# The values of the folded stage's attention blocks, two at a time instead of one by one

## The chip, the cores and the metric

The kernel runs on one core of a Trainium2 chip. A core has five engines, each with its own instruction stream: TensorE (PE in the profile), VectorE (DVE), ScalarE (ACT), GpSimd (POOL) and SyncE (SP), which here only issues loads. They meet through semaphores. The metric is the device time of one execution in microseconds, the median over the runs.

## The reference

Three stages follow each other. The first is attention over a window of 64 positions, for 4 batches, 8 heads, 576 positions and a head dimension of 64:

```python
scores = scale * np.matmul(q, k.transpose(0, 1, 3, 2))
mask = (rel >= 0) & (rel < window)
scores = np.where(mask, scores, -1000000000.0)
attn = np.exp(scores - np.max(scores, axis=-1, keepdims=True))
attn = attn / (np.sum(attn, axis=-1, keepdims=True) + 1e-09)
return np.matmul(attn, v).astype(np.float32)
```

The second is a gated product, the third a mixture of 8 experts of which each token takes the one with the largest logit:

```python
h = a * b @ w3                      # a = x @ w1, b = x @ w2
x = h @ w_out
h = np.maximum(x[mask] @ w1[e], 0.0)
out[mask] = gate_w[mask, None] * eom[mask, e, None] * (h @ w2[e])
```

## The kernel before

Products in full precision are made of three matmuls of a high and a low part of each operand (`product3`): ScalarE writes the high part of a tile, VectorE the low part, which is the difference.

**The fold.** Before any token is worked on, the kernel multiplies `w3` by `w_out` (with the gate weights beside it) into one matrix, `Wh` and `Wl`. That takes 16 steps, in the order of `w_order`. Each is 24 matmuls of 128 x 256 or 128 x 272 into one of banks 0 to 3 of PSUM. Then ScalarE copies the bank into `Wh` and VectorE puts the rest into `Wl`. The steps are numbered by `i` from 0 to 15. The code for attention counts `e = i - 2`.

**Attention blocks.** Attention is cut into blocks of three times 64 positions for four heads. The stage here called `b = 0` is the first four blocks, `p` = 0 to 3, and it is worked on between the steps of the fold. The others (`b > 0`) are worked on in the main loop, four in each chunk of 384 tokens, between its tiles. A block passes through this chain:

- `score` (TensorE, L593): 12 matmuls.
- `masks` (VectorE): scale and mask, lay out into `prob`, row maximum.
- `exps` (ScalarE): exponentials and their sums, in `prob`.
- `weigh` (VectorE) and `normal` (GpSimd, L1474): reciprocal of the sums, multiplication of `prob`. It releases `p_ok`.
- `turn` (TensorE, L609): three transposes of `prob` into a bank. It releases `pt_done`.
- `turn_out` (VectorE, L1055): four instructions for a block that copy the transposes into `pT` with the mask at the sides. They release `pt_ok`, two for a block.
- `value` (TensorE, L621): 12 matmuls of `vv` and `pT` into a bank. It releases `o_done`.
- `value_hi` (ScalarE, L850) and `value_lo` (VectorE, L1069): the result as high and low part in `xTh` and `xTl`. `value_lo` releases `o_lo`.

`prob` has two buffers and `pT` four, of which a block uses two (`buf_of`). Loads of values go into two buffers as well, and `load_v(G)` on SyncE's queue waits until block G - 2 has been multiplied (`o_done`).

**What sets the order.** Each engine runs its instructions in the order in which the program gives them. The tables `scored`, `laid`, `raised`, `weighed`, `turned` and `valued` say at which `e` a part of a block's work stands; on TensorE, `attend` puts it behind the matmuls of that step, as turns, values, scores. On VectorE a step has first its own part (`own`: weights' low parts and the step's `Wl`), then turned, valued, laid. `last_valued` are the blocks whose values stand in the middle of the last step, after its third group of matmuls. The first chunk begins when `o_lo` has counted all four blocks.

Of the kernel before, what the change touches and what calls it, by code (L numbers as in the profile page):

```python
# [37 lines left out]
def build(nc, B, H, S, qk_pairs, v_pairs, w1, w2, w3T_in, w_out, w_outT, w_gates, ew1, ew2, out):  # L38
# [35 lines left out]
    NP = len(PLACES) // STAGES  # L74
# [7 lines left out]
    with ctx:  # L82
# [131 lines left out]
        bank = [ctx.enter_context(nc.psum_tensor(f"bank{i}", [P, 512], F32)) for i in range(8)]  # L214

        def sem(name):
            return ctx.enter_context(nc.semaphore(name))
# [19 lines left out]
        pt_done, pt_ok, o_done, o_hi, o_lo = sem("pt_done"), sem("pt_ok"), sem("o_done"), sem("o_hi"), sem("o_lo")  # L237
# [31 lines left out]

        head_of_row = lambda G: PLACES[G][2] == 0  # L270
        score_bank = lambda b, p, h: bank[(4 if b > 0 and p == 1 else 5) + 2 * h]
        turn_bank = lambda b, p: bank[6 if b > 0 and p % 2 else 4]
        value_bank = lambda b, p: bank[4 if b > 0 and p % 2 else 6]
        buf_of = lambda p, h: p % 2 * 2 + h
        stats = lambda p: slice(p % 2 * 6, p % 2 * 6 + 6)

# [11 lines left out]
            return ({2: (0,), 3: (1,), 7: (2,), 9: (3,)} if b > 0 else {2: (0,), 4: (1,), 7: (2,), 10: (3,)}).get(e, ())  # L288

        def turned(b, e):  # L290
            return ({3: (0,), 4: (1,), 9: (2,), 11: (3,)} if b > 0 else {4: (0,), 7: (1,), 9: (2,), 11: (3,)}).get(e, ())

        def valued(b, e):
            return ({6: (0, 1)} if b > 0 else {7: (0,), 9: (1,), 11: (2,)}).get(e, ())

        def last_valued(b):
            return (2, 3) if b > 0 else (3,)

# [23 lines left out]
        def hidden_bank(cc, f, m):  # L324
            return bank[(2 * (cc + f) + m) % 4]
# [159 lines left out]
        def _(pe):  # L485
# [112 lines left out]

            def turn(b, p):
                G = b * NP + p  # L600
                if b == 0 and G > 0:
                    pe.wait_ge(pt_ok, 2 * G)
                if b > 0 and p < 2:
                    pe.wait_ge(masked, 2 * (b * NP + 2))
                if b > 0 and p >= 2:
                    pe.wait_ge(o_lo, b * NP + 2)
                pe.wait_ge(p_ok, G + 1)
                for i in range(3):
                    mm = pe.transpose(turn_bank(b, p)[:, i * P:(i + 1) * P], prob[p % 2][:, i * P:(i + 1) * P], ident[:, :])  # L609
                mm.then_inc(pt_done, 1)  # L610

            def value(b, p):
                G = b * NP + p
                pe.wait_ge(v_in[G % 2], 16 * (G // 2 + 1))
                pe.wait_ge(pt_ok, 2 * G + 2 if b == 0 else 2 * (b * NP + p // 2 * 2 + 2))
                if b == 0 and G > 0:
                    pe.wait_ge(o_lo, G)
                for h in range(2):
                    for i in range(3):
                        for r in range(2):  # L620
                            mm = pe.matmul(value_bank(b, p)[r * D:(r + 1) * D, (3 * h + i) * WIN:(3 * h + i + 1) * WIN],  # L621
                                           vv[G % 2][:, (i * 4 + r * 2 + h) * D:(i * 4 + r * 2 + h + 1) * D],
                                           pT[buf_of(p, h)][:, i * P + r * WIN:i * P + (r + 1) * WIN], start=True, stop=True)
                mm.then_inc(o_done, 1)
# [11 lines left out]
            for i, (it, n) in enumerate(w_order):  # L636
                if i == 0:
                    W_first_two()
                if i < 2:
                    continue  # L640
                def between(j):
                    if (i, j) == (2, 4):
                        pe.wait_ge(wg_in, 16)
                        G1_product(0)
                    if (i, j) in ((3, 0), (3, 1), (3, 3)):
                        G1_product((j + 3) // 2)
                    if (i, j) == (3, 6):
                        pe.wait_ge(const_ok, 1)
                        G1_turn()
                    if (i, j) == (len(w_order) - 1, 2):  # L650
                        for p in last_valued(0):
                            value(0, p)

                W_half(it, n, between)
                if i < len(w_order) - 1:
                    attend(0, i - 2)

            def chunk(cc, c, b, final):
                pe.wait_ge(o_lo, (cc + 1) * NP)
                pe.wait_ge(xB_ok, cc * CT + 1)  # L660
                pe.wait_ge(xA_ok, max(cc * CT - 1, 1))

                def hidden_tile(f):
                    if f < 2:
                        pe.wait_ge(W_lo, 2 * KF - 2 + 2 * f)
                        if f == 1 and cc > 0:
                            pe.wait_ge(xA_ok, cc * CT + 1)
                    else:
                        pe.wait_ge(a_ok, cc * KF + (f - 1))
                        pe.wait_ge(ab_ok, cc * KF + (f - 1))  # L670
                    for m, (wh, wl, done) in enumerate(((w1h, w1l, a_done), (w2h, w2l, b_done))):
                        for kt in range(KD):
                            if cc == 0 and f == 0:
                                pe.wait_ge(w12_lo, m * KD + kt + 1)
                            ws = slice(kt * FF + f * P, kt * FF + (f + 1) * P)
                            xc = slice(kt * SUPER + c * CH, kt * SUPER + (c + 1) * CH)
                            mm = product3(hidden_bank(cc, f, m)[:, 0:CH], wh[:, ws], wl[:, ws], xTh[:, xc], xTl[:, xc],
                                          kt == 0, kt == KD - 1)
                        mm.then_inc(done, 1)

                def row_tile(i, n, tt, between=None):
                    if i == 0:
                        pe.wait_ge(a_ok, cc * KF + (KF - 1))
                        pe.wait_ge(ab_ok, cc * KF + (KF - 1))
                    if i >= 4:
                        pe.wait_ge(xB_ok, cc * CT + (i - 2))
                    first, end = PARTS[n]
                    for f in range(KF):
                        if i == 0:
                            pe.wait_ge(ab_lo, cc * KF + (f + 1))  # L690
                        ts = slice(f * CH + tt * P, f * CH + (tt + 1) * P)
                        ws = slice(f * WXC + first, f * WXC + end)
                        mm = product3(row_bank(cc, i)[:, 0:end - first], abh[:, ts], abl[:, ts], Wh[:, ws], Wl[:, ws],
                                      f == 0, f == KF - 1)
                        if between and f == 2:
                            between()
                    mm.then_inc((xA_done, xB_done)[n], 1)

                if b is not None:
                    score(b, 0)  # L700
                    score(b, 1)
                for f in range(KF):
                    hidden_tile(f)
                    if b is not None:
                        attend(b, f)
                    if final and f == 1:
                        early_ranks()
                    if final and f == 4:
                        early_ids()
                for n, tt, i in row_tiles:  # L710
                    if b is not None and KF + i == NSTEP - 1:
                        row_tile(i, n, tt, lambda: [value(b, p) for p in last_valued(b)])
                    else:
                        row_tile(i, n, tt)
                        if b is not None:
                            attend(b, KF + i)
                    if final and i == 1:
                        x_transposes(0, bank[7])
                    if final and i == CT:
                        last_ranks()  # L720
# [115 lines left out]
        def _(act):  # L836
# [47 lines left out]
            for i, (it, n) in enumerate(w_order):  # L884
# [10 lines left out]
                                   ACT.Copy).then_inc(W_hi, 1)  # L895

                if i == len(w_order) - 1:
                    for p in last_valued(0):
                        value_hi(0, p)
                own()  # L900
                for p in valued(0, i - 2):
# [16 lines left out]
            def chunk(cc, c, b, final):  # L918
# [27 lines left out]
                                xs_out(0, bank[7])  # L946
                for n, tt, i in row_tiles:
                    if b is not None and KF + i == NSTEP - 1:
                        for p in last_valued(b):
                            value_hi(b, p)  # L950
                    row_tile(i, n, tt)
                    attend(KF + i)
# [76 lines left out]
        def _(dve):  # L1029
# [88 lines left out]
            for i, (it, n) in enumerate(w_order):  # L1118
# [25 lines left out]
                    dve.tensor_tensor(Wl[:, ws], w_bank(i)[:, 0:end - first], f32(Wh[:, ws]), ALU.subtract).then_inc(W_lo, 1)  # L1144

                if i == len(w_order) - 1:
                    for p in last_valued(0):
                        value_lo(0, p)
                own()
                attend(0, i - 2)  # L1150
# [8 lines left out]
            def chunk(cc, c, b, final):  # L1159
# [32 lines left out]
                for n, tt, i in row_tiles:  # L1192
# [4 lines left out]
                        else:  # L1197
                            xs_out(0, bank[7])
                    if b is not None and KF + i == NSTEP - 1:
                        for p in last_valued(b):  # L1200
                            value_lo(b, p)
                    row_tile(i, n, tt)
                    if b is not None:
# [389 lines left out]
```

## Time and profile before

| | |
|---|---|
| median of 3 runs | 697.99 us (697.89 to 698.15) |
| the profiled execution | 697.63 us, span 695.5 us |
| TensorE busy | 688.3 us, 99% of the span |
| VectorE busy | 367.7 us, 53% |
| ScalarE busy | 269.0 us, 39% |
| GpSimd busy | 105.9 us, 15% |
| the fold on TensorE | about 5.6 to 67.3 us |

The busy times are those of one execution, whose times in the rows count from the start of its span. The span leaves out what lies around it, about 2 us. The shares are averages over stages that differ: over the whole span VectorE has much room, but from 40 to 50 us it is busy for 9.77 of 10 us.

### The profile page before, as it was taken

What the parts mean: (1) busy time and instruction counts of PE and PEld (TensorE: products, weight loads), DVE (VectorE), ACT (ScalarE), POOL (GpSimd) and SP (SyncE); (2) the same over time, 40 slices, a digit from 0 to 9 for tenths busy, and PEclk for the clock granted to TensorE, in tenths of its full rate; (3) what the DMA queues carried; (4) which work ended last, traced back from release to release, by engine and by line L of the source; (5) the groups of instructions that cost most, each with busy time, mean ns of one, the idle gap of its engine ahead of it and who ended that gap; (6) DMA issues with size and microseconds to landing.
All of it is one profiled execution on the core that took longest, in us unless ns stands there. A gap on an engine that the chain in (4) does not pass through costs nothing.

```text
span 695.5 us, 14656 instructions
## 1 busy us (share of the span) xinstructions
PE 688.3 (99%) x5043; PEld 629.2 (90%) x5044; DVE 367.7 (53%) x696; ACT 269.0 (39%) x653; POOL 105.9 (15%) x173
## 2 busy tenths in 40 slices
PE   8999999999999999999999999999999999999997
PEld 6899999999999999999999998888888888888885
DVE  5598565355265546436535488654465634652111
ACT  5546432234143232324322255263454535542121
POOL 7110001000000100000010002222222222221111
PEclk9999999999999999999999999999999999999999
DMA  8973112302402030240125053844456554411110
GB/s 330 341 252 109 50 41 75 130 27 73 142 4 99 33 113 27 73 146 1 47 88 200 16 182 135 282 162 155 161 179 228 190 166 161 151 36 45 33 45 31
DMA packets 29917, 82.76 MB, mean 119 GB/s; under 512 B 3565, under 2 KB 3693, under 8 KB 29872
## 3 DMA queue, kind: packets, MB, share of 16 engines
q1 hardware_dynamic: 24832, 66.66, 28.1%
q0 software_dynamic: 5040, 15.47, 6.4%
q8 instruction: 32, 0.52, 0.3%
q14 instruction: 13, 0.11, 0.0%
HBM read 72.68 MB, written 10.49 MB: 120 GB/s over the span
## 4 chain that ended last, share of the span: by engine, by line
PE 96%; DMA 2%; SPq 1%; issue 0%; POOLq 0%; ACT 0%; ACTq 0%
PE bank L489 29%; PE bank L491 28%; PE bank L490 28%; PE bank L786 3%; PE bank L621 3%; PE bank L593 3%; DMA qk<-in_qk 2%; PE bank L764 1%; PE bank L609 1%; PE bank L746 1%; SPq L403 1%; SPq L390 0%; SPq L399 0%; PE bank L741 0%; POOLq L82 0%
## 5 line engine op out<-in xcount | busy, mean ns | idle before, releaser
L489 PE MATMUL bank<-Wh,abh 128*128 128x272 f32 (+1 forms) x288 | 83.5, 290 | 0.0
L491 PE MATMUL bank<-Wh,abl 128*128 128x272 f32 (+1 forms) x288 | 82.0, 285 | 0.0
L1156 DVE TENSOR_TENSOR wbuf<-raw,wbuf 128x1024 f32 (+1 forms) x64 | 75.3, 1221 | 12.5 <-ACT wbuf L915 12.4
L490 PE MATMUL bank<-Wl,abh 128*128 128x272 f32 (+1 forms) x288 | 81.7, 284 | 0.0
L1350 DVE TENSOR_TENSOR hTl<-bank,hTh 128x512 fp32r<-128x512 f32 x44 | 28.4, 686 | 97.3 <-ACT hTh L965 97.3
L1169 DVE TENSOR_TENSOR ab_f<-bank,a_sb 128x384 f32<-128x384 f32 x48 | 26.8, 558 | 90.5 <-PE bank L491 90.0
L489 PE MATMUL bank<-wbuf,hTh 128*128 (+1 forms) x176 | 70.7, 402 | 0.0
L489 PE MATMUL bank<-wbuf,xsTh 128*128 (+1 forms) x176 | 70.4, 400 | 0.0
L491 PE MATMUL bank<-wbuf,hTl 128*128 (+1 forms) x176 | 68.8, 391 | 0.0
L491 PE MATMUL bank<-wbuf,xsTl 128*128 (+1 forms) x176 | 68.6, 390 | 0.0
L490 PE MATMUL bank<-wbuf,xsTh 128*128 (+1 forms) x176 | 68.6, 390 | 0.0
L490 PE MATMUL bank<-wbuf,hTh 128*128 (+1 forms) x176 | 68.5, 389 | 0.0
L489 PE MATMUL bank<-xTh,w1h 128*128 128x384 f32 x192 | 66.5, 346 | 0.0
L491 PE MATMUL bank<-xTh,w1l 128*128 128x384 f32 x192 | 64.3, 335 | 0.0
L490 PE MATMUL bank<-xTl,w1h 128*128 128x384 f32 x192 | 64.3, 335 | 0.0
L491 PE MATMUL bank<-xTh,w2l 128*128 128x384 f32 x192 | 64.2, 334 | 0.0
L489 PE MATMUL bank<-xTh,w2h 128*128 128x384 f32 x192 | 64.1, 334 | 0.0
L490 PE MATMUL bank<-xTl,w2h 128*128 128x384 f32 x192 | 64.1, 334 | 0.0
L915 ACT ACTIVATE wbuf<-raw 128x1024 f32 (+1 forms) x64 | 64.0, 1054 | 0.0
L923 ACT ACTIVATE abh<-ab_f 128x384 fp32r<-128x384 f32 x48 | 25.2, 525 | 98.2 <-DVE ab_f L1169 98.2
L1474 POOL TENSOR_TENSOR prob<-prob,rec 128x384 f32<-128x384 f32 x24 | 21.7, 905 | 257.0 <-DVE rec L1065 257.0
L1055 DVE TENSOR_TENSOR pT<-bank,side 64x384 f32<-64x384 f32 x96 | 52.8, 550 | 14.6 <-PE bank L609 13.2
(208 smaller groups left out, 1438.1 us busy)
## 6 DMA issues: line engine op xcount, KB each, us to landing
raw<-in_expert_w SPq DMA_DIRECT2D x64, 512.0 KB, 4.4
qk<-in_qk SPq DMA_DIRECT2D x24, 448.0 KB, 4.3
vv<-in_v SPq DMA_DIRECT2D x24, 384.0 KB, 4.0
x_rows<-x_sb POOLq DMA_DIRECT2D x18, 256.0 KB, 2.3
w3r<-in_w3T SPq DMA_DIRECT2D x5, 512.0 KB, 3.6
wo<-in_w_out SPq DMA_DIRECT2D x8, 256.0 KB, 8.2
woT<-in_w_outT SPq DMA_DIRECT2D x4, 512.0 KB, 8.6
w1r<-in_w SPq DMA_DIRECT2D x4, 512.0 KB, 4.8
```

What stands on the lines that cost most here:

```text
L489: pe.matmul(dst, lh, rh, start=first, stop=False)
L490: pe.matmul(dst, lh, rl, start=False, stop=False)
L491: return pe.matmul(dst, ll, rh, start=False, stop=last)
L593: mm = pe.matmul(score_bank(b, p, h)[r * WIN:(r + 1) * WIN, i * P:(i + 1) * P], buf[rows, r * QC + i * WIN:r * QC + (i + 1) * WIN], buf[ro ...
L621: mm = pe.matmul(value_bank(b, p)[r * D:(r + 1) * D, (3 * h + i) * WIN:(3 * h + i + 1) * WIN], vv[G % 2][:, (i * 4 + r * 2 + h) * D:(i * 4 ...
L915: act.activation(wbuf[:, bass.ds(wcol(e, part, 0, c * PC), PC)], raw[part * NP1 + c][:, :], ACT.Copy).then_inc(ew_hi[part], 1)
L923: act.activation(abh[:, f * CH:(f + 1) * CH], ab_f[f % 2][:, :], ACT.Copy).then_inc(ab_hi, 1)
L1055: cut = dve.tensor_tensor(pT[buf_of(p, h)][w * WIN:(w + 1) * WIN, :].rearrange("p (i r c) -> p i r c", r=2, c=WIN), turn_bank(b, p)[rows, ...
L1156: dve.tensor_tensor(wbuf[:, bass.ds(wcol(e, part, 1, c * PC), PC)], raw[part * NP1 + c][:, :], f32(wbuf[:, bass.ds(wcol(e, part, 0, c * PC ...
L1169: dve.tensor_tensor(ab_f[f % 2][:, :], hidden_bank(cc, f, 1)[:, 0:CH], a_sb[f % 2][:, :], ALU.mult).then_inc(ab_ok, 1)
L1350: dve.tensor_tensor(hTl[last][:, cols], bank[3 + n][:, :], f32(hTh[last][:, cols]), ALU.subtract).then_inc(hT_lo, 1)
L1474: pool.tensor_tensor(pv, pv, rec[:, stats(p)].unsqueeze(2).broadcast_to([P, 6, WIN]), ALU.mult).then_inc(p_ok, 1)
```

## The change

The values of blocks 0 and 1 are both multiplied behind step 9 (`e` = 7), those of blocks 2 and 3 both in the last step. Before, they stood behind step 9, 11 and 13 and in the last step. The transposes of block 1 stand behind step 8 instead of 9. The banks of odd blocks are exchanged: their transposes go to bank 6 and their values to bank 4, as in the main loop. With that the waits change: `value` waits for the `pt_ok` of both blocks of its pair, and `turn` of blocks 2 and 3 waits for the `o_lo` of blocks 0 and 1.

```diff
-        turn_bank = lambda b, p: bank[6 if b > 0 and p % 2 else 4]
-        value_bank = lambda b, p: bank[4 if b > 0 and p % 2 else 6]
+        turn_bank = lambda b, p: bank[6 if p % 2 else 4]
+        value_bank = lambda b, p: bank[4 if p % 2 else 6]
...
         def turned(b, e):
-            return ({3: (0,), 4: (1,), 9: (2,), 11: (3,)} if b > 0 else {4: (0,), 7: (1,), 9: (2,), 11: (3,)}).get(e, ())
+            return ({3: (0,), 4: (1,), 9: (2,), 11: (3,)} if b > 0 else {4: (0,), 6: (1,), 9: (2,), 11: (3,)}).get(e, ())
 
         def valued(b, e):
-            return ({6: (0, 1)} if b > 0 else {7: (0,), 9: (1,), 11: (2,)}).get(e, ())
-
-        def last_valued(b):
-            return (2, 3) if b > 0 else (3,)
+            return {6 if b > 0 else 7: (0, 1)}.get(e, ())
+
+        last_valued = (2, 3)
...
             def turn(b, p):
                 G = b * NP + p
-                if b == 0 and G > 0:
-                    pe.wait_ge(pt_ok, 2 * G)
                 if b > 0 and p < 2:
                     pe.wait_ge(masked, 2 * (b * NP + 2))
-                if b > 0 and p >= 2:
+                if p >= 2:
                     pe.wait_ge(o_lo, b * NP + 2)
...
                 pe.wait_ge(v_in[G % 2], 16 * (G // 2 + 1))
-                pe.wait_ge(pt_ok, 2 * G + 2 if b == 0 else 2 * (b * NP + p // 2 * 2 + 2))
-                if b == 0 and G > 0:
-                    pe.wait_ge(o_lo, G)
+                pe.wait_ge(pt_ok, 2 * (b * NP + p // 2 * 2 + 2))
```

The other places of the diff take `last_valued` as a tuple instead of calling it.

TensorE at the end of step 9, before. The first row is the step's last matmul; `prob1` is block 1's probabilities, `pT0` and `pT1` are block 0's transposes.

```order
L491 MATMUL bank1<-xTl_56,w3l0_106 128x272
L609 MATMUL bank4<-ident_81,prob1_72 128x128 [waits p_ok,pt_ok]
L609 MATMUL bank4<-ident_81,prob1_72 128x128 x2
L621 MATMUL bank6<-pT0_73,vv0_68 64x64 [waits pt_ok,v_in0]
L621 MATMUL bank6<-pT0_73,vv0_68 64x64 x5
L621 MATMUL bank6<-pT1_74,vv0_68 64x64 x6
L593 MATMUL bank5<-qk1_67 64x128 [waits masked,qk_in1]
```

The same place after. `pT2` and `pT3` are block 1's transposes, `vv1` its values.

```order
L490 MATMUL bank1<-xTl_56,w3l0_106 128x272
L616 MATMUL bank6<-pT0_73,vv0_68 64x64 [waits pt_ok,v_in0]
L616 MATMUL bank6<-pT0_73,vv0_68 64x64 x5
L616 MATMUL bank6<-pT1_74,vv0_68 64x64 x6
L616 MATMUL bank4<-pT2_75,vv1_69 64x64 [waits pt_ok,v_in1]
L616 MATMUL bank4<-pT2_75,vv1_69 64x64 x5
L616 MATMUL bank4<-pT3_76,vv1_69 64x64 x6
L592 MATMUL bank5<-qk1_67 64x128 [waits masked,qk_in1]
```

Block 1's transposes have left this place and its values have come to it; the first values' `pt_ok` now counts both blocks. The transposes stand between step 8 and step 9, as follows (after):

```order
L490 MATMUL bank0<-xTl_56,w3l0_106 128x256
L606 MATMUL bank6<-ident_81,prob1_72 128x128 [waits p_ok]
L606 MATMUL bank6<-ident_81,prob1_72 128x128 x2
L488 MATMUL bank1<-xTh_55,w3h0_110 128x272 [waits g1_lo,W_lo,w3_lo]
```

VectorE around the same steps, before. The rows begin with the two low parts of weights and the `Wl` of step 8 (out of bank 0); the `Wl` out of bank 1 is that of step 9.

```order
L1076 TENSOR_TENSOR w3l2_108<-w3r2_104,w3h2_112 128x1024 [waits w3_hi]
L1083 TENSOR_TENSOR w1l_50<-w1r_115,w1h_49 128x1024 [waits w12_hi]
L1144 TENSOR_TENSOR Wl_54<-bank0,Wh_53 128x256 [waits W_hi]
L1063 TENSOR_SCALAR sums_85<-sums_85 128x6 [waits exp_ok]
L1065 RECIPROCAL rec_86<-sums_85 128x6 [waits sum_ok]
L1144 TENSOR_TENSOR Wl_54<-bank1,Wh_53 128x272 [waits W_hi]
L1055 TENSOR_TENSOR pT2_75<-bank4,side_78 64x384 [waits pt_done]
L1055 TENSOR_TENSOR pT2_75<-bank4,side_78 64x384
L1055 TENSOR_TENSOR pT3_76<-bank4,side_78 64x384 [waits pt_done]
L1055 TENSOR_TENSOR pT3_76<-bank4,side_78 64x384
L1069 TENSOR_TENSOR xTl_56<-bank6,xTh_55 128x2x192 [waits o_hi]
```

And after:

```order
L1071 TENSOR_TENSOR w3l2_108<-w3r2_104,w3h2_112 128x1024 [waits w3_hi]
L1078 TENSOR_TENSOR w1l_50<-w1r_115,w1h_49 128x1024 [waits w12_hi]
L1139 TENSOR_TENSOR Wl_54<-bank0,Wh_53 128x256 [waits W_hi]
L1050 TENSOR_TENSOR pT2_75<-bank6,side_78 64x384 [waits pt_done]
L1050 TENSOR_TENSOR pT2_75<-bank6,side_78 64x384
L1050 TENSOR_TENSOR pT3_76<-bank6,side_78 64x384 [waits pt_done]
L1050 TENSOR_TENSOR pT3_76<-bank6,side_78 64x384
L1058 TENSOR_SCALAR sums_85<-sums_85 128x6 [waits exp_ok]
L1060 RECIPROCAL rec_86<-sums_85 128x6 [waits sum_ok]
L1139 TENSOR_TENSOR Wl_54<-bank1,Wh_53 128x272 [waits W_hi]
L1064 TENSOR_TENSOR xTl_56<-bank6,xTh_55 128x2x192 [waits o_hi]
L1064 TENSOR_TENSOR xTl_56<-bank4,xTh_55 128x2x192 [waits o_hi]
```

The four copies of block 1's transposes have moved up past the sums of block 2 and past step 9's `Wl`, three instructions; what stands ahead of them is as before. The low part of block 1's values has come up from the next step but one.

## Rows read from the trace of the kernel before

**Rows 1.** The page, busy time of the engines, with share of the span and instructions.

```profile
PE 688.3 (99%) x5043; PEld 629.2 (90%) x5044; DVE 367.7 (53%) x696; ACT 269.0 (39%) x653; POOL 105.9 (15%) x173
```

**Rows 2.** TensorE's waits over the span: total us, times, longest.

```profile
PE bank L577 <- DVE prob L1099: 1.5, 1, 1.5
PE bank L593 <- DMA qk<-in_qk: 1.0, 2, 0.6
```

**Rows 3.** Timeline of TensorE in the fold: start, us, instructions merged.

```profile
43.61 0.29 PE L491 MATMUL bank<-xTl,w3l 128*128 128x272 f32 x1
43.73 0.49 PE L609 MATMUL bank<-ident,prob 128*128 128x128 f32 x3
44.16 0.92 PE L621 MATMUL bank<-pT,vv 128*64 128x64 f32 x24
45.00 0.89 PE L593 MATMUL bank<-qk 64*64 64x128 f32 x24
45.82 0.39 PE L489 MATMUL bank<-xTh,w3h 128*128 128x256 f32 x1
...
58.98 0.49 PE L609 MATMUL bank<-ident,prob 128*128 128x128 f32 x3
...
60.25 0.39 PE L489 MATMUL bank<-xTh,w3h 128*128 128x256 f32 x1
...
64.41 0.92 PE L621 MATMUL bank<-pT,vv 128*64 128x64 f32 x24
65.26 0.39 PE L489 MATMUL bank<-xTh,w3h 128*128 128x272 f32 x1
```

**Rows 4.** Timeline of TensorE in two chunks of the main loop.

```profile
112.56 0.49 PE L609 MATMUL bank<-ident,prob 128*128 128x128 f32 x3
112.81 0.37 PE L489 MATMUL bank<-Wh,abh 128*128 128x272 f32 x1
...
182.02 0.28 PE L491 MATMUL bank<-Wh,abl 128*128 128x256 f32 x1
182.22 1.62 PE L621 MATMUL bank<-pT,vv 128*64 128x64 f32 x48
183.77 0.38 PE L489 MATMUL bank<-Wh,abh 128*128 128x256 f32 x1
```

**Rows 5.** Timeline of VectorE in the fold.

```profile
40.65 1.01 DVE L1037 SCALAR_TENSOR_TENSOR sm<-bank,mask 128x384 f32<-128x384 f32 x2
...
42.76 1.22 DVE L1076 TENSOR_TENSOR w3l<-w3r,w3h 128x1024 fp32r<-128x1024 f32 x1
43.90 1.22 DVE L1083 TENSOR_TENSOR w1l<-w1r,w1h 128x1024 fp32r<-128x1024 f32 x1
45.03 0.42 DVE L1144 TENSOR_TENSOR Wl<-bank,Wh 128x256 fp32r<-128x256 f32 x1
45.36 0.16 DVE L1063 TENSOR_SCALAR sums<-sums 128x6 f32<-128x6 f32 x1
...
45.98 2.27 DVE L1055 TENSOR_TENSOR pT<-bank,side 64x384 f32<-64x384 f32 x4
```

**Rows 6.** Timelines of GpSimd and ScalarE in the fold; in brackets the idle time before.

```profile
35.43 1.73 POOL L1474 TENSOR_TENSOR prob<-prob,rec 128x384 f32<-128x384 f32 x1 [8.27 <-DVE rec L1065]
...
57.09 1.72 POOL L1474 TENSOR_TENSOR prob<-prob,rec 128x384 f32<-128x384 f32 x1 [10.42 <-DVE rec L1065]
...
53.15 0.49 ACT L850 ACTIVATE xTh<-bank 128x384 fp32r<-128x384 f32 x1 [0.79 <-PE bank L621]
```

**Rows 7.** TensorE's first and last matmuls, and a window with granted clock (PEclk).

```profile
5.60 0.77 PE L541 MATMUL bank<-xTh,w3h 128*128 128x256 f32 x2
...
8.00 0.40 PE L541 MATMUL bank<-xTh,w3h 128*128 128x256 f32 x2
...
690.40 0.39 PE L491 MATMUL bank<-wbuf,hTl 128*128 x1
...
692.00:694.00 2.00, 0.00 (x0) 0.00 (x0) 0.00 (x0) 0.00 (x0) 0.98 (x1) 0.75 0.03 12
```

More of the change, by code:

```diff
@@ L650, in between @@
                     if (i, j) == (len(w_order) - 1, 2):
-                        for p in last_valued(0):
+                        for p in last_valued:
                             value(0, p)
@@ L711, in chunk @@
                     if b is not None and KF + i == NSTEP - 1:
-                        row_tile(i, n, tt, lambda: [value(b, p) for p in last_valued(b)])
+                        row_tile(i, n, tt, lambda: [value(b, p) for p in last_valued])
                     else:
@@ L897, in _ @@
                 if i == len(w_order) - 1:
-                    for p in last_valued(0):
+                    for p in last_valued:
                         value_hi(0, p)
@@ L948, in chunk @@
                     if b is not None and KF + i == NSTEP - 1:
-                        for p in last_valued(b):
+                        for p in last_valued:
                             value_hi(b, p)
@@ L1146, in _ @@
                 if i == len(w_order) - 1:
-                    for p in last_valued(0):
+                    for p in last_valued:
                         value_lo(0, p)
@@ L1199, in chunk @@
                     if b is not None and KF + i == NSTEP - 1:
-                        for p in last_valued(b):
+                        for p in last_valued:
                             value_lo(b, p)
```

## The prediction

> **What bounds the kernel now.** I read the page first: TensorE is busy for 99% of the span [rows 1], so time is won or lost only where TensorE's own stream gets shorter or where it has to stand still. The view of waits then says how rarely it stands: 1.5 us before the first matmul and 1.0 us for two loads of queries and keys [rows 2], and nothing at all between those loads and the end of the fold. Every microsecond of waiting that the change puts into the fold therefore goes into the total, because nothing later is idle that could give it back.
>
> Next, TensorE's timeline at the places where attention work interrupts the fold. I write T for the three transposes of a block (L609), V for its values (L621), S for its scores (L593). What counts is from start to start: from the first instruction of the interruption to the next fold matmul. Step 9 ends in T, V, S of blocks 1, 0, 3: T begins at 43.73, V at 44.16, S at 45.00, the fold goes on at 45.82, so T V S costs 2.09 us, of which S is 0.82. Step 13 ends in T V, 58.98 to 60.25, 1.27 us, and step 11 in the same. The V in the last step runs from 64.41 to 65.26, 0.85 us [rows 3]. Then VectorE's timeline just ahead of step 9's end: it hands one instruction to the next without a gap from 40.65 to 45.98 [rows 5]. In this stretch VectorE is as much as two steps behind TensorE: its share of step 8, the low part of the folded matrix, starts at 45.03, when TensorE is already through step 9.
>
> **The change part by part.** *The interruptions.* The chunks of the main loop already take the new forms, so their prices are in the trace: T alone costs 0.25 us (112.56 to 112.81), and two V's together 1.55 us (182.22 to 183.77), behind a lead of 0.20 us where 0.12 is usual (43.61 to 43.73), 0.08 more [rows 3, 4]. Before: 2.09 + 1.27 + 1.27 + (0.85 + 0.08) = 5.56 us. After: T behind step 8 0.25, V V S behind step 9 0.08 + 1.55 + 0.82 = 2.45, T behind steps 11 and 13 0.25 each, V V in the last step 1.63, together 4.83 us. The arrangement saves 0.73 us of TensorE's time. The work is the same; what goes is changes between kinds of matmuls.
>
> The Trainium skill (TensorEngine Tiling (Array Packing), its list of constraints) says that a change of the tiling mode drains TensorE. The saving above has that sign, and by that rule alone the change would be a small gain.
>
> *T of block 1, one step sooner.* Its probabilities are ready: GpSimd's multiplication for it starts at 35.43 and takes 1.73 us, to 37.16 [rows 6], and step 8 ends near 40.7 (step 9's 24 matmuls, 0.12 us apart, end at 43.73). So T itself waits for nothing.
>
> *V of block 0, now with block 1.* Its wait on `pt_ok` was for block 0 alone; now it is for both blocks. Block 1's transposes are copied out by VectorE in four instructions of together 2.27 us [rows 5]. In VectorE's order these now stand right behind the low part of step 8 and ahead of the two small operations at 45.36 and of step 9's low part. What is ahead of them is unchanged and has no gap: scores' mask at 40.65, two splits at 42.76 and 43.90, the low part at 45.03, next start 45.36 [rows 5]. None of it waits for TensorE's later work, so moving T forward does not make VectorE come sooner. The copies run from 45.36 to 45.36 + 2.27 = 47.63. TensorE is ready for V V at 43.73 + 0.25 (the T put in behind step 8) + 0.08 = 44.06. It waits 47.63 − 44.06 = 3.57 us. Before, V of block 0 needed only copies that were long done, and block 1's copies were covered by two more steps, 10 and 11. That cover is gone. Queued behind the waiting V on TensorE are V of block 1, S of block 3 and all of steps 10 to 15, and every other engine ends up waiting for these.
>
> Sum of the fold: 3.57 − 0.73 = +2.84 us.
>
> *What is late next.* T of block 2 now waits for both low parts of the values (`o_lo`), which VectorE does some 2.5 us after V V begins; two whole steps lie between. T of block 3 is the closest one: now its probabilities are ready at 57.09 + 1.72 = 58.81, and T starts at 58.98, 0.17 us later [rows 3, 6]. After the change T of block 3 comes 3.57 + (0.25 + 2.45 − 2.09) − (1.27 − 0.25) = 3.16 us later. The chain to the probabilities starts from step 11's end, later by 3.57 + 0.61 = 4.18, but ScalarE loses the copy of block 1's values from it, 0.79 us of waiting and some 0.4 us of work [rows 6]; that makes about 3.0. The margin stays, thin. I cost it at nothing, with up to 1 us as its bad end. V V in the last step wants block 3's copies, 2.3 us of VectorE behind T; there the last V came five microseconds behind T and V V comes one microsecond sooner, so some margin is left. The loads of values are issued in pairs now; the one that moves later is used in the middle of the first chunk, tens of microseconds on. Nothing.
>
> *The clock of TensorE after the wait.* No row of before shows a wait like this inside the kernel. The nearest rows: the last matmul starts at 690.40 and takes 0.39 us, and the granted clock averages 0.75 in 692 to 694, half of it at 2.4 GHz and half at 1.2; it fell about 2.2 us after the last matmul [rows 7]. A wait of 3.57 us is longer than that, so I expect the lower level behind it. What that costs is bounded by the beginning: from the first matmul at 1.5 us [rows 2], two 256-column matmuls still take 0.77 us at 5.60 and only 0.40 us at 8.00 [rows 7] (the clock record itself reads 1.00 there; the durations say half). So the return took 4.1 to 6.5 us, and half of that, 2.0 to 3.2 us, is lost. Below, the bound is 0, if the clock doesn't fall or is back at once. I take the middle of 0 to 3.2, 1.6 us.
>
> The Trainium skill (TensorE: Matmul & The Clock Gate, "What's actually happening") says that the lower clock is the default and that activity lifts it. By that rule a stall is paid for twice, which is the term that I add; without it the sum would be 1.6 us less.
>
> Total: 2.84 + 1.6 = +4.44 us. The profiled execution took 697.63 us (span 695.5), which gives 702.1; the median of the runs is 0.36 us above it, which gives 697.99 + 4.44 = **702.4 us**.
>
> **The rivals.**
> *The wait without the clock.* Same stall, clock stays at 2.4 GHz: 697.99 + 2.84 = 700.8 us. For it: after the last matmul the clock held for 2.2 us, and when it falls may differ from place to place. Against it: the wait is longer by more than a microsecond. 22%.
> *VectorE is in time (the other side).* Then only the regrouping counts: 697.99 − 0.73 = 697.3 us, not slower. It needs the copies to start by 44.06 − 2.27 = 41.8 us, 3.6 us sooner than 45.36; this decides it. For it only that ScalarE and the loads might release VectorE's earlier work sooner; against it, the chain in [rows 5] has no gap from 40.65 on that could close. 6%.
> *A shorter wait.* The copies start partly sooner, TensorE waits some 2 us or less and keeps its clock: 697.99 + 2 − 0.73 = 699.3 us. 5%.
> *More than one wait, or a long stay at the low clock.* The probabilities of block 3 are late as well, by up to 1 us, or the low clock costs its full 3.2 us: 703.4 to 704.0 us, both together 705.0. The margin of 0.17 us speaks for it, the shorter chain on ScalarE against it. 9%.
>
> **How the numbers follow.** My forecast, the wait with the clock's fall at about 1.6 us, has 58%. With the wait alone (22%) that is 80%; the range from 700.3 to 703.9 us takes in both, the clock term's spread and nearly all of the long stay. A measurement of this kernel tells about 0.2% (1.4 us) from no change. Faster by more than that needs a mechanism that no row shows: 2%. Within it lie VectorE in time and a part of the shorter wait: 8%. Slower: 90%.
>
> **What the profile after would show.** In VectorE's timeline the four copies at about 45.4 to 47.6, ahead of the sums of block 2. In the view of waits a line of TensorE's V waiting for VectorE's pT, about 3.6 us, once; this is the step on which all rests. V V behind step 9 and in the last step at about 1.55 us each, if the clock is up; behind step 9 nearer to 3 us, and the next fold matmuls 0.21 to 0.25 us apart in place of 0.12, if it fell; the granted clock of 48 to 52 us well below 1. T of block 3 without a wait. The first chunk starting about 4.4 us later (2.8 if the clock held), and from there the same distance between all rows of before and after. I am wrong if VectorE reaches the copies early, if the clock stays up, or if a second wait shows in steps 12 to 15.

## The result, and the profile after

The changed kernel takes 702.58 us (median of 6 runs, 701.9 to 704.15) beside 697.94 us (median of 6, 697.38 to 698.2) for the kernel before: ratio 1.0072, 95% interval 1.0061 to 1.0082. It is 4.64 us slower. The profiled execution took 702.89 us with a span of 700.8 us. Three executions in all that follows ran far slower than every other of their kernel (879.93 and 973.4 us of the kernel before, 1380.4 us in one experiment); they are left out of the ratios and move the medians below by at most 0.07 us.

Busy time, share and instructions by engine, after, from the page:

```profile
PE 689.2 (98%) x5043; PEld 630.1 (90%) x5044; DVE 368.7 (53%) x696; ACT 269.2 (38%) x653; POOL 105.9 (15%) x173
```

The work is that of [rows 1]; only the span around it is longer. TensorE's waits over the span, after (total us, times, longest):

```profile
PE bank L616 <- DVE pT L1050: 3.5, 1, 3.5
PE bank L592 <- DMA qk<-in_qk: 1.6, 2, 1.3
PE bank L576 <- DVE prob L1094: 1.5, 1, 1.5
```

The first line is new; the other two are those of [rows 2], the loads' with 0.6 us more in this execution. TensorE's values wait once, for the copies of the transposes. Its timeline there, after, from the T behind step 8 to the end of step 10, and further below T V V S in the rest of the fold (L606 is T, L616 V, L592 S, L488 to L490 the fold):

```profile
41.39 0.49 PE L606 MATMUL bank<-ident,prob 128*128 128x128 f32 x3
41.63 0.37 PE L488 MATMUL bank<-xTh,w3h 128*128 128x272 f32 x1
...
44.59 0.28 PE L490 MATMUL bank<-xTl,w3l 128*128 128x272 f32 x1
48.41 1.76 PE L616 MATMUL bank<-pT,vv 128*64 128x64 f32 x48 [3.54 <-DVE pT L1050]
50.10 1.56 PE L592 MATMUL bank<-qk 64*64 64x128 f32 x24
51.59 0.58 PE L488 MATMUL bank<-xTh,w3h 128*128 128x256 f32 x1
...
52.19 0.41 PE L490 MATMUL bank<-xTh,w3l 128*128 128x256 f32 x1
52.40 0.41 PE L488 MATMUL bank<-xTh,w3h 128*128 128x256 f32 x1
...
53.34 0.28 PE L490 MATMUL bank<-xTh,w3l 128*128 128x256 f32 x1
53.46 0.28 PE L488 MATMUL bank<-xTh,w3h 128*128 128x256 f32 x1
...
55.21 0.29 PE L488 MATMUL bank<-xTh,w3h 128*128 128x272 f32 x1
...
58.47 0.36 PE L488 MATMUL bank<-xTh,w3h 128*128 128x256 f32 x1
...
61.41 0.29 PE L488 MATMUL bank<-xTh,w3h 128*128 128x272 f32 x1
...
64.43 0.49 PE L606 MATMUL bank<-ident,prob 128*128 128x128 f32 x3
64.67 0.36 PE L488 MATMUL bank<-xTh,w3h 128*128 128x256 f32 x1
...
68.84 1.62 PE L616 MATMUL bank<-pT,vv 128*64 128x64 f32 x48
70.39 0.39 PE L488 MATMUL bank<-xTh,w3h 128*128 128x272 f32 x1
```

VectorE in the same stretch, after:

```profile
41.29 1.01 DVE L1032 SCALAR_TENSOR_TENSOR sm<-bank,mask 128x384 f32<-128x384 f32 x2
...
43.40 1.22 DVE L1071 TENSOR_TENSOR w3l<-w3r,w3h 128x1024 fp32r<-128x1024 f32 x1
44.53 1.22 DVE L1078 TENSOR_TENSOR w1l<-w1r,w1h 128x1024 fp32r<-128x1024 f32 x1
45.67 0.42 DVE L1139 TENSOR_TENSOR Wl<-bank,Wh 128x256 fp32r<-128x256 f32 x1
46.00 2.27 DVE L1050 TENSOR_TENSOR pT<-bank,side 64x384 f32<-64x384 f32 x4
48.30 0.17 DVE L1058 TENSOR_SCALAR sums<-sums 128x6 f32<-128x6 f32 x1
```

And the engines' busy times and granted clock (PEclk, third number from the end) in windows, after:

```profile
46.00:48.00 2.00, 0.00 (x0) 0.00 (x0) 1.94 (x5) 0.00 (x0) 0.00 (x0) 1.00 0.66 242
48.00:50.00 2.00, 1.58 (x48) 1.60 (x48) 1.18 (x5) 0.49 (x1) 0.83 (x1) 0.94 0.00 0
50.00:52.00 2.00, 2.00 (x29) 1.57 (x27) 1.26 (x3) 1.44 (x2) 0.00 (x0) 0.50 0.68 197
52.00:54.00 2.00, 2.00 (x14) 2.00 (x14) 0.97 (x1) 0.00 (x0) 0.00 (x0) 0.71 0.58 159
```

How to read these against the rows of before. VectorE does the same work in the same order up to 45.67, as in [rows 5], only 0.64 us later, because the fold itself began later behind the loads. From 46.00 to 48.27 it copies block 1's transposes. TensorE could have begun the pair at 44.59 + 0.20 = 44.79 and begins it at 48.41: 3.62 us. Then the pair takes 1.69 us (48.41 to 50.10) where it takes 1.55 in [rows 4], the scores 1.49 (50.10 to 51.59) where they took 0.82 in [rows 3], and step 10 takes 3.62 (51.59 to 55.21) where step 12, of the same 24 matmuls, takes 2.94 (58.47 to 61.41). That is 0.14 + 0.67 + 0.68 = 1.49 us for the clock. It is still at 2.4 GHz through the wait and for the first 1.3 us of the pair, then at 1.2 GHz from about 49.7 to about 53.2. The sum: 3.62 + 1.49 − 0.73 = 4.38 us, and with 0.6 us more for the loads 5.0 of the 5.3 us by which the two spans differ. The first chunk starts at 73.94 us where it started at 68.82, 5.1 us later, and the last matmul at 695.66 instead of 690.40, 5.3 us later: nothing behind the fold gave time back.

### The profile page after: what moved, and what is told of

Same layout as the page of the kernel before. It is cut to its first block, busy times and chain, and to the rows that moved or that the text cites. A ratio compares the mean times of both kernels' runs of the same rounds, so it can differ in the third digit from the quotient of the medians.

```text
span 700.8 us, 14655 instructions
## 1 busy us (share of the span) xinstructions
PE 689.2 (98%) x5043; PEld 630.1 (90%) x5044; DVE 368.7 (53%) x696; ACT 269.2 (38%) x653; POOL 105.9 (15%) x173
## 4 chain that ended last, share of the span: by engine, by line
PE 93%; DMA 2%; DVE 2%; SPq 1%; ACT 1%; issue 0%; POOLq 0%; ACTq 0%
PE bank L488 28%; PE bank L490 27%; PE bank L489 27%; PE bank L781 3%; PE bank L616 3%; PE bank L592 3%; DMA qk<-in_qk 2%; PE bank L759 1%; PE bank L606 1%; DVE pT L1050 1%; DMA w3r<-in_w3T 1%; PE bank L741 1%; SPq L402 0%; SPq L389 0%; DVE w3l L1071 0%
## 5 line engine op out<-in xcount | busy, mean ns | idle before, releaser
L488 PE MATMUL bank<-Wh,abh 128*128 128x272 f32 (+1 forms) x288 | 83.5, 290 | 0.0
L490 PE MATMUL bank<-Wh,abl 128*128 128x272 f32 (+1 forms) x288 | 82.0, 285 | 0.0
L488 PE MATMUL bank<-wbuf,hTh 128*128 (+1 forms) x176 | 70.7, 402 | 0.1
L488 PE MATMUL bank<-wbuf,xsTh 128*128 (+1 forms) x176 | 70.4, 400 | 0.0
L490 PE MATMUL bank<-wbuf,hTl 128*128 (+1 forms) x176 | 68.8, 391 | 0.0
L490 PE MATMUL bank<-wbuf,xsTl 128*128 (+1 forms) x176 | 68.6, 390 | 0.0
L488 PE MATMUL bank<-xTh,w1h 128*128 128x384 f32 x192 | 66.5, 346 | 0.0
L490 PE MATMUL bank<-xTh,w1l 128*128 128x384 f32 x192 | 64.3, 335 | 0.0
L490 PE MATMUL bank<-xTh,w2l 128*128 128x384 f32 x192 | 64.2, 334 | 0.0
L488 PE MATMUL bank<-xTh,w2h 128*128 128x384 f32 x192 | 64.1, 334 | 0.0
```

Of the source, the lines that this page charges most:

```text
L488: pe.matmul(dst, lh, rh, start=first, stop=False)
L490: return pe.matmul(dst, ll, rh, start=False, stop=last)
```

## The experiments

All are compared with the kernel before on the same chip; ratios carry their 95% interval. First, does the wait alone make the loss, and is it VectorE's order that sets it?

**The wait without the regrouping.** The kernel before with one number changed:

```diff
-                pe.wait_ge(pt_ok, 2 * G + 2 if b == 0 else 2 * (b * NP + p // 2 * 2 + 2))
+                pe.wait_ge(pt_ok, max(2 * G + 2, 4) if b == 0 else 2 * (b * NP + p // 2 * 2 + 2))
```

> The kernel before with one number changed: the values of block 0 behind step 9 wait for the copies of both blocks, as in the changed kernel; grouping, banks and order are those of before. Theory of the late copies: the transposes of block 1 are issued just ahead, VectorE's copies end at about 48.3 us where TensorE is ready at 44.2, a wait of 4.1 us, and the clock falls behind it for about 1.6 us: 697.9 + 5.7 = 703.6 us. Rival, the loss comes from the regrouping: this kernel then stays within 1 us of the kernel before.

Measured: 703.82 us (703.47 to 704.1, 5 runs) beside 698.17, ratio 1.0078 (1.0065 to 1.0092). Its wait and clock:

```profile
PE bank L621 <- DVE pT L1055: 4.1, 1, 4.1
```

```profile
48.00:50.00 2.00, 0.52 (x10) 0.55 (x12) 1.28 (x3) 0.00 (x0) 0.00 (x0) 0.83 0.00 0
50.00:52.00 2.00, 2.00 (x40) 1.88 (x40) 0.42 (x1) 0.94 (x2) 0.00 (x0) 0.50 0.00 0
```

The one added wait makes a loss of 5.6 us, with nothing regrouped: 4.1 us of waiting, and 1.45 us of clock (from its first V to step 11 it takes 6.03 us, 49.48 to 55.51, where the kernel before takes 4.58, 44.16 to 48.74). Wait and time are what was expected.

**The copies first on VectorE.** The changed kernel; block 1's copies stand ahead of step 8's own part:

```diff
                 def own():
+                    if i == 8:
+                        turn_out(0, 1, 0)
+                        turn_out(0, 1, 1)
                     for p in weighed(0, i - 2):
...
                 for p in turned(b, e):
+                    if b == 0 and p == 1:
+                        continue
                     turn_out(b, p, 0)
```

> The changed kernel, but VectorE copies block 1's transposes as its first work of step 8, ahead of the two low parts of weights and of step 8's own low part (2.6 us of work in the profile). Theory of the late copies: they end 2.6 us sooner, TensorE's wait shrinks from 3.6 to about 1.0 us, and a wait of 1 us leaves the clock up: 697.9 - 0.7 + 1.0 = 698.2 us. Rival, the wait comes from the transposes or from their probabilities (TensorE, GpSimd), not from VectorE's order: wait and time as in the changed kernel, 702.6 us.

Measured: 698.69 us (median of 12 runs) beside 698.17, ratio 1.0004 (0.9995 to 1.0013). The copies now run from 43.69, and the pair starts at 46.10:

```profile
43.69 2.27 DVE L1050 TENSOR_TENSOR pT<-bank,side 64x384 f32<-64x384 f32 x4
45.98 1.23 DVE L1071 TENSOR_TENSOR w3l<-w3r,w3h 128x1024 fp32r<-128x1024 f32 x1
```

```profile
PE bank L616 <- DVE pT L1050: 1.1, 1, 1.1
```

The granted clock stays at 1.00. So it is VectorE's queue that sets the wait: 2.6 us of work moved behind the copies shortens it by 2.4 us, from 3.5 to 1.1. The time is 0.5 us above what was expected.

**The pair one step later.** The changed kernel with one number changed:

```diff
-            return {6 if b > 0 else 7: (0, 1)}.get(e, ())
+            return {6 if b > 0 else 8: (0, 1)}.get(e, ())
```

> The changed kernel with the pair of blocks 0 and 1 multiplied one step later, behind step 10 instead of 9. Theory of the late copies (VectorE reaches block 1's copies only at about 46.0 us and ends them at 48.3, TensorE waits for them): TensorE comes to the pair at about 49.4 us by the clock of the profiled run, so the wait is 0, the clock stays at its upper level, and what is left is the regrouping, -0.7 us: 697.2 us, ratio 0.999. Rival, the pairing and the exchanged banks themselves cost something (waits for o_lo, more work in one piece): the time stays at 700 us or above although the copies are in time.

Measured: 697.39 us (697.07 to 697.91, 11 runs) beside 698.17, ratio 0.9989 (0.9980 to 0.9998). The copies end at 47.97, the pair starts at 48.35, 0.20 us behind the last matmul of step 10, the lead of [rows 4]:

```profile
45.70 2.27 DVE L1050 TENSOR_TENSOR pT<-bank,side 64x384 f32<-64x384 f32 x4
```

```profile
48.15 0.27 PE L490 MATMUL bank<-xTl,w3l 128*128 128x256 f32 x1
48.35 1.62 PE L616 MATMUL bank<-pT,vv 128*64 128x64 f32 x48
```

No wait of TensorE for VectorE is left. What is left is the regrouping alone, −0.78 us where −0.73 was worked out. On another chip, once more:

> The changed kernel with the first pair behind step 10, once more on another chip, to see whether its small gain holds: -0.7 us by the regrouping, ratio about 0.999, no wait of TensorE for VectorE. Rival: the first measurement's -0.8 us was chance, and it is not to be told from the kernel before.

Measured: 697.22 us (696.52 to 698.78, 11 runs) beside 698.05, ratio 0.9992 (0.9983 to 1.0001). The medians differ by 0.83 us, but here the interval reaches 1. The gain was found twice at nearly the same size and is at the edge of what can be told. This is the best version.

**Which half of the change.** Each half was put into the kernel before alone, with the banks and waits that it needs (left out here). The first:

```diff
-            return ({3: (0,), 4: (1,), 9: (2,), 11: (3,)} if b > 0 else {4: (0,), 7: (1,), 9: (2,), 11: (3,)}).get(e, ())
+            return ({3: (0,), 4: (1,), 9: (2,), 11: (3,)} if b > 0 else {4: (0,), 6: (1,), 9: (2,), 11: (3,)}).get(e, ())
...
-            return ({6: (0, 1)} if b > 0 else {7: (0,), 9: (1,), 11: (2,)}).get(e, ())
+            return ({6: (0, 1)} if b > 0 else {7: (0, 1), 11: (2,)}).get(e, ())
```

> The kernel before with one half of the change: the values of blocks 0 and 1 together behind step 9, block 1's transposes behind step 8; blocks 2 and 3 as before. Theory of the late copies: all of the loss is here, wait 3.6 us and clock 1.6 us, less 0.4 us of regrouping: 702.7 us. Rival, the loss is shared by both halves: 700 to 701 us.

Measured: 702.12 us (700.54 to 704.0, 6 runs) beside 698.27, ratio 1.0059 (1.0044 to 1.0073), and the wait of the changed kernel:

```profile
PE bank L623 <- DVE pT L1057: 3.5, 1, 3.5
```

The second:

```diff
-            return ({6: (0, 1)} if b > 0 else {7: (0,), 9: (1,), 11: (2,)}).get(e, ())
+            return ({6: (0, 1)} if b > 0 else {7: (0,), 9: (1,)}).get(e, ())
...
-            return (2, 3) if b > 0 else (3,)
+            return (2, 3)
```

> The kernel before with the other half of the change: the values of blocks 2 and 3 are multiplied together in the last step (with the banks exchanged for block 3); blocks 0 and 1 are as before. Theory of the late copies: this half has time enough on VectorE, no wait, and its share of the regrouping is what remains: before 1.27 + 0.93, after 0.25 + 1.63, so -0.3 us, 697.6 us, same within the measurement. Rival, this half brings a wait of its own (block 3's copies late in the last step): 1 to 2 us more, 699 to 700 us.

Measured: 697.74 us (697.01 to 698.36, 11 runs) beside 698.27, ratio 0.9994 (0.9985 to 1.0003), and no wait for VectorE. The loss is in the first pair; the second costs nothing.

**The transposes back behind step 9.** The changed kernel with one entry undone:

```diff
-            return ({3: (0,), 4: (1,), 9: (2,), 11: (3,)} if b > 0 else {4: (0,), 6: (1,), 9: (2,), 11: (3,)}).get(e, ())
+            return ({3: (0,), 4: (1,), 9: (2,), 11: (3,)} if b > 0 else {4: (0,), 7: (1,), 9: (2,), 11: (3,)}).get(e, ())
```

> The changed kernel with one part undone: block 1's transposes stand behind step 9 again, just ahead of the pair, and no longer behind step 8. Theory of the late copies: on VectorE the copies then stand behind step 9's low part again and end 0.6 us later, at about 48.25 us in the times of before; TensorE would be ready at 44.2, so the wait grows from 3.6 to about 4.1 us, while one interruption fewer gives nearly nothing; with the clock's fall 702.6 + 0.4 = 703.0 us. Rival, the sooner transposes are what costs: the time falls toward 698 us.

Measured: 703.28 us (702.99 to 704.55, 5 runs) beside 698.17, ratio 1.0076 (1.0062 to 1.0089). The median is near the 703.0 us expected; the changed kernel itself, run beside it on the same chip (below), has 701.94, so the difference there is 1.3 us where 0.4 was expected. The profiled execution was the slowest, 704.55 us, and waits longer than I had said:

```profile
PE bank L616 <- DVE pT L1050: 5.1, 1, 5.1
```

The extra microsecond does not come from the edit. In this execution ScalarE waited longer for a weight tile's load early in the fold:

```profile
32.95 1.06 ACT L851 ACTIVATE w3h<-w3r 128x1024 fp32r<-128x1024 f32 x1 [1.72 <-DMA w3r<-in_w3T]
```

In the changed kernel the same instruction starts at 32.51, after 0.78 us; in the kernel before, at 31.88. So beside the kernel before it is 1.07 us late, while TensorE reaches the transposes behind step 9 only 0.16 us late (43.89 against 43.73). That load comes well ahead of the place of the edit. Behind the weight tile stand block 1's exponentials, and VectorE waits for these before its long row of work without a gap (after):

```profile
35.60 0.17 DVE L1058 TENSOR_SCALAR sums<-sums 128x6 f32<-128x6 f32 x1 [2.81 <-ACT prob L840]
```

That gave a new question: is VectorE's lag made there?

**The exponentials ahead of the weight tile.** The changed kernel; on ScalarE, step 5 does `exps` of block 1 first and then `hi_w3`:

```diff
-                if i in w3_steps:
+                if i in w3_steps and i != 5:
                     hi_w3(w3_steps[i])
...
                 for p in raised(0, i - 2):
                     exps(0, p)
+                if i == 5:
+                    hi_w3(w3_steps[i])
```

> The changed kernel with two pieces of ScalarE's step 5 exchanged: block 1's exponentials come ahead of the high part of a weight tile, whose load they waited behind (0.8 us in the profile of before, 1.7 us in that of the kernel with the later transposes). Theory of the late copies, one step further back: VectorE's lag begins where it waits for these exponentials at 32 to 35 us and is then carried without a gap to block 1's copies. VectorE goes on about 1.1 us sooner, the wait shrinks from 3.3 to 3.6 us to about 2.4 us, and the time by 1.1 us or, where the clock then stays up, by 2.8 us: 699.8 to 701.5 us. Rival, the lag arises later (step 7's mask and splits alone): wait and time as in the changed kernel.

Measured: 701.04 us (699.65 to 702.49, 7 runs) beside 698.05, ratio 1.0035 (1.0024 to 1.0046).

```profile
33.75 0.17 DVE L1060 TENSOR_SCALAR sums<-sums 128x6 f32<-128x6 f32 x1 [0.97 <-ACT prob L840]
...
45.03 2.27 DVE L1052 TENSOR_TENSOR pT<-bank,side 64x384 f32<-64x384 f32 x4
```

```profile
PE bank L616 <- DVE pT L1052: 2.6, 1, 2.6
```

VectorE goes on 1.85 us sooner, waits 0.6 us once more for the weight tile, and reaches the copies at 45.03 in place of 46.00. TensorE's wait is 2.6 us in place of 3.5. The time is 1.5 us below the changed kernel's 702.58, and 0.9 us below the 701.94 of its repetition. So about 1 us of VectorE's lag at step 8 begins at step 5, on ScalarE behind a load; the other 2.6 us don't, and no run here traces them further back.

Last, the clock.

**Matmuls in place of the wait.** The changed kernel with 26 extra matmuls behind step 9, whose results nobody uses:

```diff
+                if (b, e) == (0, 7):
+                    pe.wait_ge(W_lo, 7)
+                    for _ in range(26):
+                        pe.matmul(bank[2][:, 0:DM // 2], wol[:, 0:P], wol[:, 0:DM // 2], start=True, stop=True)
                 for p in valued(b, e):
```

> The changed kernel with 26 extra matmuls of 128 x 256 (about 3.1 us at the upper clock; their results are not used) just ahead of the pair behind step 9, in the place of most of the wait. The copies still end at the same time. Theory of the clock (1.5 to 1.7 us of the loss come from TensorE's clock falling behind the wait): the copies are waited for as before, but the clock stays at 2.4 GHz, 702.6 - 1.6 = about 701.0 us, and the granted clock reads 1.00 from 48 to 54 us. Rival, the clock is no part of the loss: 702.6 us or more.

Measured: 701.23 us (700.62 to 702.64, 5 runs) beside 698.17, ratio 1.0042 (1.0028 to 1.0055).

```profile
44.42 3.27 PE L627 MATMUL bank<-wol 128*128 128x256 f32 x26
48.38 1.62 PE L616 MATMUL bank<-pT,vv 128*64 128x64 f32 x48 [0.69 <-DVE pT L1054]
49.92 0.89 PE L592 MATMUL bank<-qk 64*64 64x128 f32 x24
...
53.67 0.29 PE L488 MATMUL bank<-xTh,w3h 128*128 128x272 f32 x1
```

```profile
50.00:52.00 2.00, 2.00 (x34) 1.83 (x35) 1.40 (x3) 1.44 (x2) 0.00 (x0) 1.00 0.78 208
```

The pair starts at 48.38, in the changed kernel at 48.41, and the clock stays at 1.00. From the start of the pair to the start of step 11, the same matmuls take 5.29 us (48.38 to 53.67) where they took 6.80 (48.41 to 55.21): with TensorE kept at work through most of the delay, 1.51 us come back, the size of the 1.49 us found above. The clock is a term of its own. The medians alone show it less sharply: 701.23 is 1.35 us below the changed kernel's 702.58, but only 0.7 us below the 701.94 of its repetition. The profiled execution was the slowest of the five; it has a wait of 0.7 us for a load of token rows far behind the fold, which neither the profile before nor the one after has; whether the edit has a part in it is not shown.

**The changed kernel once more**, for its single times:

> The changed kernel itself, once more on this chip beside another. If the clock's fall comes at a point that differs from execution to execution, its single times lie at more than one level, some 1.7 us apart, between 700.9 (no fall) and 704.2 us, where those of the kernel before stay within 1 us; if the fall is bound to the wait they lie together at 702.6 us.

Measured: 700.14, 701.67, 701.94, 702.43 and 702.65 us, ratio 1.0049 (1.0035 to 1.0062) to 698.17; those of before on this chip lie from 697.64 to 698.64. The 700.14 us run has a mean granted clock of 1.000 over its span (the five lie from 0.994 to 1.000), so there the clock can hardly have fallen; it was not the profiled one. In the profiled one (702.65) it fell during the wait and cost more than in the first profile:

```profile
46.00:48.00 2.00, 0.48 (x9) 0.51 (x11) 1.86 (x6) 0.00 (x0) 0.12 (x1) 0.62 0.45 180
48.00:50.00 2.00, 2.00 (x44) 2.00 (x41) 0.64 (x2) 0.49 (x1) 0.71 (x1) 0.50 0.00 0
50.00:52.00 2.00, 2.00 (x32) 1.55 (x30) 0.82 (x3) 1.43 (x2) 0.00 (x0) 0.50 0.69 197
52.00:54.00 2.00, 2.00 (x13) 2.00 (x14) 1.15 (x1) 0.00 (x0) 0.00 (x0) 0.67 0.52 152
```

```profile
47.52 2.83 PE L616 MATMUL bank<-pT,vv 128*64 128x64 f32 x48 [3.33 <-DVE pT L1050]
...
55.38 0.29 PE L488 MATMUL bank<-xTh,w3h 128*128 128x272 f32 x1
```

From the pair to step 11 it is 7.86 us (47.52 to 55.38), 2.57 us more than with the matmuls filled in. Measured the same way, the first half of the change lost 2.52 us to the clock, the late transposes 2.03 and the exponentials first 1.52. So the clock's part differs from execution to execution, as the theory that its fall comes at a differing point has it. The single times spread, rather than falling into clean levels.

## Why the prediction was right

**The bound.** That a wait in the fold is never given back held: the first chunk starts 5.1 us late and the last matmul 5.3 us late.

**The interruptions.** −0.73 us was the sum from the rows of the chunks. The pair behind step 10 leaves just this term and measures −0.78 and −0.83 us. In the trace after, T alone takes 0.24 us (41.39 to 41.63, 64.43 to 64.67) and the undisturbed V V 1.55 (68.84 to 70.39).

**The wait.** Predicted 47.63 − 44.06 = 3.57 us, measured 3.62. The four copies stand where the order put them and take the 2.27 us of [rows 5]. The claim that moving T forward doesn't bring VectorE sooner fits the experiment with the late transposes: its median is 0.7 us above the changed kernel's (1.3 us on the same chip), of which some 0.6 us are the three small instructions that stand ahead of the copies there.

**What is late next.** Nothing. Block 3's probabilities are ready at 62.26 + 1.73 = 63.99 us and its T starts at 64.43: the margin grew from 0.17 us to 0.44. In the last step the copies end at 65.79 + 2.27 = 68.06 and V V starts at 68.84.

```profile
62.26 1.73 POOL L1469 TENSOR_TENSOR prob<-prob,rec 128x384 f32<-128x384 f32 x1 [12.65 <-DVE rec L1060]
```

**The clock.** I took 1.6 us, the middle of 0 to 3.2; the profile shows 1.49, the filled wait 1.51. That the clock falls because of the wait is right. That the number came out so close is luck: it was the middle of a wide range, and over the six profiles with such a wait the term measures 1.45 to 2.57 us.

Where it falls was not predicted well. I had read a fall 2.2 us after the last matmul, which would be inside the wait, and expected the pair nearer to 3 us; in the profile of the result the clock held for some 4.9 us after the last matmul, 1.3 us into the pair, and the pair takes 1.69. In three other profiles it fell inside the wait and the pair takes 2.76 or 2.77 us.

By the windows of the result it could have been at most 1.7 us: 2 us each at 0.94, 0.50 and 0.71 of the clock lose 0.12, 1.00 and 0.58 us. My upper bound from the beginning of the kernel, 3.2 us, was wide; the 2.57 us of the later profile come nearest to it. The total has luck in it too: the changed kernel is 4.64 us above the kernel before in the first measurement and 3.77 us in the second, on either side of the 4.44 forecast. That it can fail to fall at all, which I had as a rival, occurs in single runs: 700.14 us, 1.97 us above the 698.17 of the kernel before, is even below that rival's 2.84.

**The rivals.** VectorE in time would have needed the copies by 41.8 us; they began at 46.00. What stood behind that rival, that ScalarE or a load might release VectorE's earlier work sooner, turned out to be real, but worth only about 1 us: the wait is between 3.3 and 5.1 us over five profiles (the changed kernel twice, its first half, the wait alone, the late transposes; in the last two the copies stand three small instructions, 0.6 us, further back), and 2.6 us with the exponentials first.

Open stays how much of the spread between single runs is the load's time and how much the clock's; both vary, and only profiled runs tell them apart. Open stays too what decides whether the clock falls inside the wait, behind it or not at all.

## What to carry to other kernels

Before two pieces of work are joined, look for the slowest engine in the chain to the later one, and read from its timeline when its queue reaches that piece, not when its input is ready: here the transposes were there at about 41.9 us and the queue at 46.0. A busy share of 53% over the span says nothing about this; in this stretch VectorE was full and two steps behind. A joined pair belongs behind the step at which the later half is ready anyway (here one number further on), and a stall of TensorE is to be counted with what its clock loses behind it.

## What the runs showed of the hardware

TensorE's granted clock fell to the lower level behind or inside waits of 2.6 to 5.1 us in all six profiles that have one (the changed kernel twice, its first half, the wait alone, the late transposes, the exponentials first), and cost 1.45 to 2.57 us each time. It stayed at the upper level behind waits of 1.1 us and 0.7 us. At the lower level 256-column matmuls start 0.21 us apart (52.19 to 52.40) and at the upper one 0.12 (53.34 to 53.46). By the mean granted clock of 1.000 in the 700.14 us run it doesn't fall in every execution of the same kernel. A stalled kernel's times spread more (700.14 to 704.15 us over 11 runs) than those of the kernel before (697.32 to 698.7 in all but four, the two far slower ones aside); that the clock is a cause of this is argued, not shown apart from the load's time.

The price of a switch between kinds of matmuls is seen from the two pairings: the fold is left for the values twice instead of four times, and is interrupted once more in all; together that is worth 0.7 to 0.8 us. The Trainium skill (TensorEngine Tiling (Array Packing), Key Properties, the list that the prediction means) says that a change of mode drains TensorE; the sign agrees, and the number here is the sum of the rows, not a drain measured by itself.
